# Two FFN layers behind sink attention: probabilities as the stationary operand, and GpSimd splitting output weights

## The reference

```python
scores = scale * np.matmul(q, k.transpose(0, 1, 3, 2))
scores = np.where(is_sink | in_window, scores, -1e9)
scores = scores - np.max(scores, axis=-1, keepdims=True)
a = np.exp(scores)
a = a / (np.sum(a, axis=-1, keepdims=True) + 1e-09)
x = np.matmul(a, v)                        # then (B*S, H*D) = (1536, 512)
h = x @ w_in;  x = np.maximum(0.01 * h, h) @ w_out        # w_in 512x2048
h = x @ w_in2; y = (h * (1.0 / (1.0 + np.exp(-h)))) @ w_out2
```

## Time and profile before

| | |
|---|---|
| median of 3 runs | 687.84 us (686.56 to 688.43) |
| the profiled execution | 690.34 us, span of the trace 688.4 us |
| TensorE busy | 634.6 us (92%), 3368 matmuls, each with a weight load |
| VectorE busy | 326.2 us (47%) |
| ScalarE busy | 325.9 us (47%) |
| GpSimd busy | 92.2 us (13%) |
| DMA | 57.52 MB, mean 84 GB/s |
| granted TensorE clock | mean 0.975 of full |

### The profile page before, as it was taken

How to read it: one execution, slowest core, us unless ns; L and a number is a source line. 1 busy time by engine, 2 the same in 40 slices (tenths; PEclk the granted TensorE clock), 3 DMA queues, 4 the chain that set the end, 5 groups by cost and what they waited for, 6 DMA issues and landing times.

```text
span 688.4 us, 9721 instructions
## 1 busy us (share of the span) xinstructions
PE 634.6 (92%) x3368; PEld 546.0 (79%) x3368; DVE 326.2 (47%) x780; ACT 325.9 (47%) x764; POOL 92.2 (13%) x117
## 2 busy tenths in 40 slices
PE   3649798979988999999999999999999999999997
PEld 3549798878887788888788888888888888888886
DVE  4786787746865666675322224333212322122321
ACT  5576677656765566664333336433323333223331
POOL 6341232222230322220000000000000000000000
PEclk9768999999999999999999999999999999999999
DMA  6643535413433213111002221323310112111001
GB/s 169 173 137 114 166 123 153 127 31 113 135 93 109 63 53 110 55 62 62 0 31 70 79 66 64 120 92 99 106 72 31 62 62 67 69 48 62 31 0 62
DMA packets 18096, 57.52 MB, mean 84 GB/s; under 512 B 2688, under 2 KB 2688, under 8 KB 18048
## 3 DMA queue, kind: packets, MB, share of 16 engines
q1 hardware_dynamic: 18048, 56.89, 26.9%
HBM read 53.74 MB, written 3.15 MB: 83 GB/s over the span
## 4 chain that ended last, share of the span: by engine, by line
PE 77%; DVE 10%; issue 5%; ACT 5%; DMA 1%; POOL 1%; SPq 0%; ACTq 0%; DVEq 0%; POOLq 0%
PE y_ps L841 34%; PE h_ps L810 33%; PE o_ps L774 3%; DVE sm L572 2%; PE y_ps L810 2%; PE t_ps L752 2%; PE s_ps L738 2%; DVE prob L646 2%; DVE x L593 1%; DMA qk_raw<-qk 1%; DVE win L599 1%; ACT pT L467 1%; DVE pT L582 1%; ACT q_st L447 1%; ACT win L479 1%
## 5 line engine op out<-in xcount | busy, mean ns | idle before, releaser
L810 PE MATMUL h_ps<-x,win 128*128 128x512 f32 (+1 forms) x1152 | 263.3, 374 | 6.1 <-DVE x L593 6.1
L810 PEld LDWEIGHTS h_ps<-x,win 128*128 128x128 f32 x1152 | 204.8, 190 | 42.4 <-issue 6.7
L610 DVE TENSOR_TENSOR g<-g_f,g 128x512 fp32r<-128x512 f32 (+1 forms) x112 | 72.4, 646 | 282.3 <-ACT g L494 282.3
L492 ACT ACTIVATE g_f<-h_ps 128x512 f32<-128x512 f32 (+1 forms) x96 | 53.9, 561 | 235.9 <-PE h_ps L810 235.6
L841 PE MATMUL y_ps<-g,wout 128*128 128x256 f32 (+1 forms) x768 | 153.6, 342 | 1.2 <-PE o_ps L774 0.9
L841 PE MATMUL y_ps<-wout,g 128*128 128x512 f32 x576 | 138.2, 389 | 0.0
L841 PEld LDWEIGHTS y_ps<-g,wout 128*128 128x128 f32 x768 | 120.9, 191 | 15.2 <-issue 1.5
L841 PEld LDWEIGHTS y_ps<-wout,g 128*128 128x128 f32 x576 | 108.1, 188 | 22.5
L436 ACT ACTIVATE prob<-sm,neg_max 128x260 f32<-128x260 f32 (+1 forms) x96 | 47.2, 491 | 65.5 <-DVE neg_max L572 64.8
L738 PE MATMUL s_ps<-k_hl,q_st 128*128 128x260 f32 (+1 forms) x162 | 35.8, 304 | 29.7 <-DVE neg_max L572 20.5
L599 DVE TENSOR_TENSOR win<-w_raw,win 128x512 fp32r<-128x512 f32 x72 | 53.5, 743 | 8.8 <-ACT win L479 8.4
(11 more groups left out here) (70 smaller groups left out, 428.0 us busy)
## 6 DMA issues: line engine op xcount, KB each, us to landing
w_raw<-w SPq DMA_DIRECT2D x72, 512.0 KB, 3.3
qk_raw<-qk SPq DMA_DIRECT2D x48, 260.0 KB, 4.7
v_raw<-vt SPq DMA_DIRECT2D x12, 256.0 KB, 2.6
y<-qk_raw SPq DMA_DIRECT2D x12, 256.0 KB, 2.2
vs_raw<-vsink SPq DMA_DIRECT2D x8, 8.0 KB, 2.3
```

The lines of the kernel that those rows point to most:

```text
L492: nc.scalar.activation(g_f32[:, g_at(F)], h_of(F), func, alpha=slope)
L610: nc.vector.tensor_tensor(g[:, 1, g_at(F)], g_f32[:, g_at(F)], g[:, 0, g_at(F)].bitcast(F32), ALU.subtract).then_inc(g_ready, 1)
L810: ins = mm(h_of(F), win[:, split_slot[split_of[F]], wp, c * P:(c + 1) * P], x[:, xp, c, tokens(F)], start=(c == 0 and wp == HI and xp == H ...
```

## The change

- The value product is turned round: the transposed probabilities of one head are the stationary operand (128 columns), the values of that head the moving one (64 columns). It gives queries x features, 12 matmuls of 64 columns a pair in place of 6 of 256. The result of a whole tile stands in one bank.
- Probabilities are no longer scaled. VectorE inverts a tile's eight row sums (`invert_sums`) and scales the tile's result out of its bank into `att`; TensorE transposes `att` (four 128x128), ScalarE and VectorE split that into `x`. Sinks are one transpose and one product of 512 columns a tile.
- Odd scores from a = 11 on go to another bank (`y_ps[2]`, later `y_ps[0]`), except in step B1 = 20 and from B2 = 36 on, where they go to `s_ps`.
- FFN steps: two in each of steps 11 to 17, one in each from 18 on (before: one, one, two, ... up to step 34). FFN step 16 stands in step 20, 32 in step 36 (before 23 and 35).
- The high parts of the first 16 output weight slices are made by GpSimd, behind its other work of a step. The first two weight slices are loaded at the start, the next two in steps 4 and 6; the sink values are prepared in step 7, not 5.

The core of the diff:

```diff
-        n = (1, 1, 2)[(a - FS) % 3] if F < N_NARROW else 1
-        for _ in range(n):
+        for _ in range(2 if F < FT - 2 else 1):
...
-        lead = 0 if F == FT - 1 else 2 if F + 2 < N_NARROW else 1
+        lead = 2 if F + 2 < N_NARROW and F not in (FT - 2, FT - 1, FT) else 1
...
-    sinks_of = {2 * e + 3: e for e in range(NPAIR // 2) if has_sinks(e // 2)}
+    sinks_of = {PAIRS * T + 5: T for T in range(TILES) if has_sinks(T)}
+    x_of = {PAIRS * T + 6: T for T in range(TILES)}
...
         def s_bank(n):
+            a = n // 2
             if n < S_FOUR:
                 return (s_ps, h_ps, y_ps[0], y_ps[1])[n % 4]
-            return (s_ps, y_ps[0], y_ps[1])[n % 3] if n < S_THREE else s_ps
+            if n < S_THREE:
+                return (s_ps, y_ps[0], y_ps[1])[n % 3]
+            if n % 2 == 0 or a == B1 or a >= B2:
+                return s_ps
+            return y_ps[2] if a < B1 else y_ps[0]
...
-        def o_bank(e):
-            return y_ps[3] if e < E_EARLY and e % 2 else o_ps
+        def o_bank(T):
+            return y_ps[3] if T < T_EARLY and T % 2 else o_ps
...
             load_v(0)
+            load_w(0)
+            load_w(1)
...
-                if 1 <= a <= RING:
-                    load_w(a - 1)
+                if a in (4, 6):
+                    load_w(a // 2)
...
+            def high_wout(j):
+                pool.wait_ge(w_loaded[j % RING], 16 * (j // RING + 1))
+                wait(pool, y_done, slot_left[j] + 1)
+                nc.gpsimd.tensor_copy(wout[:, split_slot[j], 0, :], w_raw[:, j % RING, HD:2 * HD]).then_inc(wout_high, 1)
...
+                for F in [u - FS] if u < FS else ticks_of[u]:
+                    for s in wout_in.get(F, ()):
+                        if s < FT:
+                            high_wout(s)
...
-                                     accum_out=row_sum[:, n % PR:n % PR + 1]).then_inc(exp_done, 1)
+                                     accum_out=row_sum[:, T % 2, h:h + 1]).then_inc(exp_done, 1)
...
+                else:
+                    dst = x[:, 0, :, i * P:(i + 1) * P]
+                    src = t_bank(k)[:, :].rearrange("p (c n) -> p c n", c=C)
...
-            def high_x(e):
-                act.wait_ge(o_done, e + 1)
-                for lo in (0, D):
-                    dst, src = attended(e, lo, 0)
-                    ins = nc.scalar.activation(dst, src, ACT.Copy)
-                ins.then_inc(x_high, 1)
...
+                if j < FT:
+                    return
+                wait(act, wout_high, FT if j == FT else 0)
...
+                if a == FS:
+                    for G in made_in[-1]:
+                        take_hidden(G)
...
+                    evacuate(F - 1, 1)
+                    for G in made_in[F] if F >= 0 else ():
+                        take_hidden(G)
+                    if n == 0 and FS < a < NPAIR:
+                        exp(2 * a + 1)
...
+                else:
+                    cols = slice(i * P, (i + 1) * P)
+                    ins = nc.vector.tensor_tensor(x[:, 1, :, cols], bank_[:, :].rearrange("p (c n) -> p c n", c=C),
+                                                  x[:, 0, :, cols].bitcast(F32), ALU.subtract)
...
-                    dst, src = attended(e, lo, 1)
-                    ins = nc.vector.tensor_tensor(dst, src, attended(e, lo, 0)[0].bitcast(F32), ALU.subtract)
...
-            def normalise(u):
-                W = width(u // PAIRS)
-                dve.wait_ge(exp_done, 2 * u + 2)
-                at = (2 * u) % PR
-                nc.vector.tensor_scalar_add(row_inv[:, u % 2, 0, :], row_sum[:, at:at + 2],
-                                            1e-9).then_inc(norm_step, 1)
-                dve.wait_ge(norm_step, 2 * u + 1)
-                nc.vector.reciprocal(row_inv[:, u % 2, 1, :], row_inv[:, u % 2, 0, :]).then_inc(norm_step, 1)
-                dve.wait_ge(norm_step, 2 * u + 2)
-                for i in range(2):
-                    a = prob[:, at + i, 0:W]
-                    nc.vector.tensor_scalar(a, a, row_inv[:, u % 2, 1, i:i + 1], None,
-                                            ALU.mult).then_inc(prob_ready, 1)
+            def invert_sums(T):
+                dve.wait_ge(exp_done, (T + 1) * H)
+                nc.vector.tensor_scalar_add(row_inv[:, 0, :], row_sum[:, T % 2, :], 1e-9).then_inc(norm_step, 1)
+                dve.wait_ge(norm_step, 2 * T + 1)
+                wait(dve, att_ready, T)
+                nc.vector.reciprocal(row_inv[:, 1, :], row_inv[:, 0, :]).then_inc(norm_step, 1)
+            def normalise(T):
+                dve.wait_ge(o_done, T + 1)
+                dve.wait_ge(norm_step, 2 * T + 2)
+                if T:
+                    dve.wait_ge(t_written, job["x", T - 1] + 1)
+                nc.vector.tensor_tensor(att[:, :].rearrange("p (h d) -> p h d", h=H),
+                                        o_bank(T)[:, :].rearrange("p (h d) -> p h d", h=H),
+                                        row_inv[:, 1, :].unsqueeze(2).to_broadcast([P, H, D]),
+                                        ALU.mult).then_inc(att_ready, 1)
...
-                if a == 5:
...
+                if a == 7:
                     stack_sink_values()
...
+                else:
+                    pe.wait_ge(att_ready, i + 1)
+                    for c in range(C):
+                        cols = slice(c * P, (c + 1) * P)
+                        ins = nc.tensor.transpose(bank_[:, cols], att[:, cols], ident[:, :])
...
-                if u % 2 == 0:
-                    wait(pe, x_ready, freed(o_bank, e))
+                if p == 0:
+                    wait(pe, att_ready, freed(o_bank, T))
                 only = not has_sinks(T)
                 slots = (0,) if width(T) == P else (0, 1)
-                for s in slots:
-                    for vp, pp in PASSES:
-                        ins = mm(pair_out(u), v_hl[:, s, vp, p * P:(p + 1) * P],
-                                 pT[:, u % 2, pp, s * 2 * P:(s + 1) * 2 * P],
-                                 start=(u % 2 == 0 and s == 0 and vp == HI and pp == HI),
-                                 stop=only and s == slots[-1] and vp == LO, skip_group_check=True)
+                for i in range(2):
+                    h = 2 * p + i
+                    for s in slots:
+                        for pp, vp in PASSES:
+                            to = s * 2 * P + i * P
+                            ins = mm(o_bank(T)[:, h * D:(h + 1) * D], pT[:, u % 2, pp, to:to + P],
+                                     v_hl[:, s, vp, h * D:(h + 1) * D],
+                                     start=(h == 0 and s == 0 and vp == HI and pp == HI),
+                                     stop=only and s == slots[-1] and pp == LO, skip_group_check=True)
                 ins.then_inc(pv_done, 1)
-                if only and u % 2:
+                if only and p == PAIRS - 1:
                     pe.wait_ge(pv_done, u + 1)
                     pe.sem_inc(o_done, 1)
-            def weigh_sinks(e):
-                T = e // 2
-                pe.wait_ge(t_ready, job["sinks", e] + 1)
-                if e == 2 * 2:
+            def weigh_sinks(T):
+                pe.wait_ge(t_ready, job["sinks", T] + 1)
+                if T == 2:
                     pe.wait_ge(vs_step, 5 + B)
-                for u in (2 * e, 2 * e + 1):
-                    p = u % PAIRS
-                    values = vs_st[:, T // TPB, 2 * p:2 * p + 2, :].rearrange("p h d -> p (h d)")
-                    ins = mm(pair_out(u), values, psT[:, :].unsqueeze(1).to_broadcast([P, 2, P]),
-                             start=False, stop=True, skip_group_check=True)
-                ins.then_inc(o_done, 1)
+                mm(o_bank(T)[:, :], psT[:, :], vs_st[:, T // TPB, :, :].rearrange("p h d -> p (h d)"),
+                   start=False, stop=True, skip_group_check=True).then_inc(o_done, 1)
...
-                        pe.wait_ge(x_ready, 2 * tokens(F).stop // P)
+                        pe.wait_ge(t_ready, job["x", tokens(F).stop // P - 1] + 1)
```

More of the change, by code:

```diff
@@ L526, in _ @@
                     exp(2 * a)
-                    if head:
+                    if a <= FS:
                         exp(2 * a + 1)
-                if head and x_half is not None:
-                    high_x(x_half)
+                if a == FS:
+                    for G in made_in[-1]:
+                        take_hidden(G)
+                if a in sinks_of:
+                    high("sinks", sinks_of[a])
+                if not head and a in x_of and a <= NPAIR:
+                    high("pair", a - 1)
                 if head and j == j_split(T):
@@ L851, in _ @@
                         scores(n)
-                    if a == FS - 1:
-                        for G in made_in[-1]:
-                            hidden(G, 0)
-                            hidden(G, 1)
-                elif a < NPAIR:
-                    scores(2 * a)
-                ticks = ticks_of[a]
```

(41 more changed lines are left out.)

118 lines of the change are left out of this document (52 added, 66 removed).

## The result

| | before | after |
|---|---|---|
| median | 687.39 us (4 runs, 686.56 to 688.43) | 715.79 us (4 runs, 714.58 to 716.50) |
| span of the profiled execution | 688.4 | 714.7 |

The ratio is 1.0411 [1.0388, 1.0433]: 28.4 us slower. The forecast was 700, 684 to 714: the sign was right, the size was not, and the time lies outside the range.

What follows compares the result with a forecast made beforehand. TensorE was taken as bound by its products in the last stretch, with 36.5 us of waits in the middle. Work +22.7, waits -11.0 and head +1.0 gave +12.7 us: 700 us, range 684 to 714.

Steps and rivals of the forecast that it cites:

- The value products: From the first FFN product on: 444 products at 0.11 us, paced by weight loads, 48.8 us for 26.0, so +22.8.
- TensorE's work: After 51.9 us: value products, sinks, attended-tile transposes and work moved ahead together add 22.7 us.
- The wait of the earlier trace: Middle stretch: TensorE's 17.9 us in 13 waits for VectorE to clear the one score bank would be nearly gone.
- Step 20's wait: Late read of block 0's second half holds bank y1: one wait of 4 us, 4.5 with step 19.
- The steps from 21 to 35: One FFN step each, ScalarE and single banks waited for: 0.5 us a step, 7.5, plus 1 for the block change.
- rival C: GpSimd's queue costs more: split steps lose 2 us more each, one-step steps 1.2; 715 or so; chance 0.14.
- Rival B: Columns, not loads, pace the value products, 0.03 to 0.06 us each: 665 to 678 us; chance 0.05.
- steps 12 to 17: Two FFN steps each, TensorE-bound: 2.5 us of slack, plus 7.5 for waiting behind GpSimd's queue from step 14.
- D: The two halves cancel: 11 to 16 us of waits kept, time within 2 us of before; chance 0.08.
- GpSimd beside VectorE: Sixteen more copies can hold VectorE up to 0.7 us each, 11 us in all; none charged beyond step 14.
- The head: Before the first FFN product: earlier loads against sink preparation, copies and tile 1's path; net +1.0 us, bounds -4 and +5.
- Rival A: Steps 11 to 35: waits fall further than work rises, 10 us kept instead of 25.5, 685 us; chance 0.18.

Runs made afterwards that it cites:

- e3: Changed kernel with value products of 128 columns in place of 64, same count and weight loads (result mixes heads): 712.98 us, 1.0364 of before.
- e4: Changed kernel with only the high x high value products, the two with low parts left out: 690.67 us, 1.0026 of before.
- e2: Changed kernel with GpSimd's output weight copies ahead of its query/key subtractions in each step: 701.76 us, 1.0195 of before.
- E6: Kernel before with only the 16 output weight copies moved from ScalarE to GpSimd, behind its other work of a step: 707.14 us, 1.0272.
- E5: As e2, with the sink values prepared in step 5 instead of step 7: 698.12 us, 1.0144 of before.
- e9: As E5, and in step 20 ScalarE and VectorE read block 0's second half out of its bank first: 693.13 us, 1.0084 of before.
- e7: Kernel before with a second bank for odd scores of steps 11 to 34, transposes keeping one bank from step 11: 687.04 us, 0.9985.
- e8: As e7, with the first 16 output weight copies made by GpSimd, not ScalarE, ahead of its query/key subtractions: 687.78 us, 0.9997 of before.
- e1: Changed kernel with the 16 output weight copies back on ScalarE, all else as changed: 706.35 us, 1.0271 of before.

## Why the prediction was wrong

**Right.** The value products: 0.11 us forecast, 0.105 in the chain, load and not columns (e3, e4). TensorE's work, 22.7 forecast and 21.5 measured, was the largest term and holds; steps 36 to 46 are 7.6 us longer together. The wait of the earlier trace rows went. Step 20's wait came with 4.0 us and step 15's with 5.9 (forecast 4 and about 6), at the places and with the releasers named. The steps from 21 to 35 lose 7.3 us (forecast 7.5 + 1), not rival C's 1.2 each. That sum is luck in part: the forecast had 0.5 in every step, but nine of the fifteen lose less than 0.1, and 6.1 us stand in steps 30, 33, 34 and 35. Rival B is refuted by e3.

By the forecast's own terms the waits are: first products at half clock 2.5, measured 2.8; steps 12 to 17, 2.5 + 7.5 = 10.0, measured 17.2; steps 19 and 20, 4.5, measured 8.3 with step 18; steps 21 to 35, 8.5, measured 7.3. Together 25.5 and 35.6. Three sums of the forecast do not come out of their terms: the head's give +1.4 and not +1.0, rival C's 8 + 10 on 700.5 give 718.5 and not 715, and 16 us of waits kept, in D, would be 3 us slower and not within 2.

**The step that failed most** is "GpSimd beside VectorE", with its sentence "so I charge none beyond step 14". The queue cost 14.0 us (e2), not 7.5: step 15 lost 10.1, since the half clock behind the wait lasted 10.2 us and cost about 4 where I had put 1.5, and steps 13 and 17 lost 4.0 and 2.1, of which 3.3 and 1.5 go with the copies: in steps 12 and 16 these stand behind the split of the tile's second half. I had followed GpSimd's order at step 14 alone. E6 is the stronger proof, since it needs none of the redesign: 18.9 us for those copies alone.

**The head** was the second: +1.0 forecast, +5.8 measured. The earlier loads did bring step 7's mask forward, from 33.9 to 29.9 us, 4 us and so more than I gave them. Steps 7 to 8 then took 10.3 us instead of 4.0. E5 prices the sink values in step 7 at 2.8 of it ("about a microsecond" in the forecast); 2.1 of that is that their two multiplications take 3.35 beside GpSimd instead of 1.29. E2 prices the copies at 1.3. What is left, 1.6, reads in e5 as follows, against the kernel before: step 7's mask comes 4.9 us earlier; steps 7 to 8 take 7.2 instead of 4.0, with VectorE idle 2.40 us for ScalarE's part of tile 0's `x` and 1.87 for its weight part; steps 8 to 10 take 1.2 less; and the path through tile 1, from step 10's mask to the first FFN product, takes 7.8 against 3.2, so 4.6 more where I had 3.2.

**Step 20** was put at 4.5 with step 19; steps 18 to 20 lost 8.3. The wait had the size forecast; again the half clock behind it (3.4 us) and 2.5 us in steps 18 and 19 were not in the sum.

**Rival C** had the time (715, by a sum that does not give it) and half of the mechanism. The steps that it named, with a split before them, are those that paid, but 1.3 to 10.1 us each and not 2, and the one-step steps paid nothing. A copy takes 0.76 us and not 1.3: it was the queue, not the length of the copies.

**Rival A** was nearer than it looks: without these three placements the waits are 15.3 us (e9), below my 25.5 and close to its 10. The redesign as e9 orders it removes 21 us of waits and adds 21.5 us of work, and its first FFN product comes 2.8 us later: 3 us slower by the profiled spans (691.4 and 688.4). So in this order it does not pay; whether another order would is open. The three placements cost the 22.7 us between 715.8 and 693.1: 14.0 GpSimd's queue, 3.6 the sink values, 5.0 the read of one bank, by medians taken apart, whose times of before lie between 687.35 and 688.26. The score bank is hardly what removes the waits: e7 gains nothing in all, and 2 us where the bank is truly added. That it is VectorE's lighter load, 326 to 272 us in all, with the new order of steps, removes them is argued from what is left and was not run by itself.

## What to carry to other kernels

Work that is moved to an idle engine must be placed by what waits ahead of it in that engine's queue: 16 copies cost nothing measurable ahead of a waiting subtraction (e8) and 18.9 us behind it (e6). Before a named wait is priced as a gain, ask what its releaser was itself waiting for; if that stays, the wait mostly moves (e7: 8.6 us of waits, 2 us of time). In this kernel a matmul with its own 128x128 weight load takes 0.105 to 0.12 us for 64 to 260 columns, so turning a product round to save columns saves nothing when it doubles the count.

## What the runs showed of the hardware

- **The clock after a wait.** With the waits of 5.9 and 4.0 us came 10.2 and 3.4 us at a granted clock of 0.5, and 3.4 us more at 84.3 us in step 13, after its waits for weights and transposes (0.34 and 1.58). With the waits gone (e9) no such stretch is left between 58 and 689 us. By the steps' losses step 15's wait was thus paid 1.7 times.
- **Half speed at the end of the head.** The changed kernel's first 24 FFN products still run at half speed (timeline of TensorE):
```profile
57.68 2.90 PE L828 MATMUL h_ps<-x,win 128*128 128x256 f32 x12 [1.22 <-DVE x L604]
60.37 2.76 PE L828 MATMUL y_ps<-x,win 128*128 128x256 f32 x12
62.93 2.01 PE L828 MATMUL h_ps<-x,win 128*128 128x256 f32 x12
64.78 1.42 PE L797 MATMUL o_ps<-v_hl,pT 128*128 128x64 f32 x12
```
  The windows say 1.00 for that stretch: the clock's first record in this trace is at 63.9 us, and what lies before it is shown as full. The distance of starts, 0.22 us a product against 0.12, tells the truth.
- **Two engines on one memory.** VectorE's subtractions take 1.06 to 1.09 us beside GpSimd's copies and 0.69 alone, GpSimd's sink copy 0.67 beside VectorE and 0.21 alone. The Trainium skill (SBUF — State Buffer, "Terms") has them exclude each other for a whole instruction, which would lay up to the copies' 12 us on VectorE, an estimate by that rule. The trace agrees in kind and not in size; VectorE's busy time, in which such blocking counts, is 269.6 us with the copies on ScalarE (e1), 270.6 in the changed kernel and 273.7 in e2, so 1 to 4 us were paid.
